# A fused attention and feed-forward kernel: first pair's queries and keys in two sets, one transfer for a pair's value windows, later feed-forward weight loads

## The chip, the cores and the metric

The kernel runs on one core of one Trainium2 chip. The metric is the device time of one execution in microseconds (us); less is better. Three runs of the kernel before took 882.73, 882.87 and 884.77 us, median 882.87 us.

## The reference

Inputs are q, k, v of shape (4, 8, 576, 64) and two pairs of feed-forward weights, (512, 2048) and (2048, 512), with two scalars s and b.

```python
# attention, per batch and head; scale = 1/8, factor = 4
q_d, k_d, v_d = means over groups of 4 positions            # 144 positions
out_d   = softmax(scale * q_d @ k_d.T) @ v_d, each row repeated 4 times
mask    = abs(pos_i - pos_j) < 4                            # band of 7
out_loc = softmax(where(mask, scale * q @ k.T, -1e9)) @ v
x = (out_d repeated + out_loc), laid out as (2304 tokens, 512)
# layer 1: h = x @ w_in;  g = h if h > 0 else exp(h) - 1;  x = g @ w_out
# layer 2: h = x @ w_in;  g = s * relu(h)**2 + b;          out = g @ w_out
```

## The kernel before, in words

The program has two stages: attention over 16 pairs of heads (four batches, four pairs `u` in each; pairs are numbered 0 to 15 below), and two feed-forward layers of 24 slots each. Each engine has its program written out in order, and semaphores join them.

**Attention.** Four buffers (slots) hold the inputs of four pairs. `qbd` holds the queries of a pair block-diagonally: head 0 in partitions 0 to 63, head 1 in 64 to 127, and zeros in the other half, which are written once. `kall` holds the keys. `vwin` holds the values as nine overlapping windows of 70 rows, one for each tile of 64 queries; `v4` holds them by groups of four positions for the pooled branch. For a pair,

- TensorE (PE) computes `scores` (L475: nine tiles of 64 queries against their windows of 70 keys, two heads, 18 products; tiles 0 to 4 go to one PSUM bank and 5 to 8 to another), `dscores` (L484, pooled), `turn` in four groups (L499 and L503, transposes of the probabilities) and `values` (L519 band, L528 pooled).
- VectorE (DVE) computes `pool_k` (L923), `mask` (L930, scale and add the band, one instruction for each bank), `max_band` (L938), `max_pooled` (L943, L947), the two `normalise` steps (L954, L956, L965, L973), and adds the two branches into `xy` (L1100).
- ScalarE (ACT) computes the exponentials (`exp_band` L674, tile by tile; `exp_pooled` L684), and copies the transposes (L761 to L771) and the pooled result (L781) out of PSUM. It zeroes the padding of slots 1 to 3 at the start (L744; slot 0 is done by DVE, L916).
- GpSimd (POOL) builds the identity and the band mask, then does `pool_q` (L434, L436) and `pool_v` (L441, L443).
- SyncE (SP) issues every DMA. `load_qk` issues one DMA for the keys (L289) and two for the queries (L293); `load_v` issues six for `vwin` (L300 to L305) and one for `v4` (L306).

The engines' programs are software-pipelined. On PE a step `i` runs `dscores(i+1)`, the first two groups of `turn(i)`, `scores(i+2)`, the last two groups, `values(i)`. On DVE the order ahead of the loop is `pool_k(0)`, `mask(0)`, `max_band(0)`, `pool_k(1)`, `max_pooled(0)`, `mask(1)`, `max_band(1)`, `normalise_band(0)`, `normalise_pooled(0)`. On POOL a step `i` waits for the probabilities of pair `i+1` and runs `pool_q(i+3)` and `pool_v(i+1)`. On SP a step `i` loads the queries and keys of pair `i+4` when pair `i` has been read, then the values of pair `i+3` when `values_ready` has counted `i+1` (it starts at 1, so the values of pair `i-1` are done). The helper `pairs` runs the first two batches as a hardware loop of four pairs and writes the last two out. `left` counts down to 0 over the pairs that are written out: in the kernel before, the first weights of the feed-forward layers (512 KB each, into `wstage`) are issued at pairs 11 (`left == 4`), 12 and 13.

**Feed-forward.** 48 slots, each of three-term products of split fp32 operands: into `ps_h` (L552 for the first two slots, L603 for the others) and into `ps_y` (L632 in layer 1, L639 in layer 2). The first product `tile(0, 0)` stands before the values of pair 15 on PE. ACT and DVE split the operands (L714, L995 for the first weights) and evaluate the activation.

Of the kernel before, what the change touches and what calls it, by code (L numbers as in the profile page):

```python
# [18 lines left out]
ALU = mybir.AluOpType  # L19
# [3 lines left out]
AX_X = mybir.AxisListType.X  # L23
# [1 line left out]
P = 128  # L25


def attention_moe_moe2(nc, q_t, k_t, v, w_in0, w_out0, w_in1, w_out1, s, b, out):
    B, H, D, S = q_t.shape
    TOK, DM = out.shape  # L30
    POOL = 4
# [13 lines left out]
    SCALE = float(D) ** -0.5  # L45
# [30 lines left out]
    RAW = (0, 1) + tuple(range(2, FP)) + (FP + 2, FP + 3) + tuple(range(NB * FP, (NB + 1) * FP))  # L76
    FETCHED = tuple(sl for sl in range(SLOTS) if sl not in RAW)

    NV = 7
    E_CREDIT = 2  # L80

    with ExitStack() as whole:
        def sem(name):
            return whole.enter_context(nc.semaphore(name))
# [57 lines left out]
        k_loaded = [sem(f"k_loaded{i}") for i in range(CH)]  # L142
        v_loaded = [sem(f"v_loaded{i}") for i in range(CH)]
        w_loaded = [[sem(f"w_{x}_loaded{i}") for i in range(2)] for x in ("in", "out")]
        sb_loaded = sem("sb_loaded")

        pads_zero = sem("pads_zero")
        slots_zero = sem("slots_zero")
        consts_ready = sem("consts_ready")
        pool_order = sem("pool_order")  # L150
        dve_order = sem("dve_order")
# [46 lines left out]

        def pairs(eng, body):

            with eng.Fori(0, B - 2) as n:
                for u in range(CH):
                    body(n, u, PAIRS)
            for n in range(B - 2, B):
                for u in range(CH):
                    body(n, u, PAIRS - 1 - (n * CH + u))

# [79 lines left out]
        def _(sp):  # L287
            def load_qk(bb, slot):
                sp.dma_start(kall[:, slot, :],  # L289
                             k_t[bb, 2 * slot:2 * slot + 2].rearrange("h d s -> (h d) s")).then_inc(k_loaded[slot], 16)  # L290
                for h in range(2):
                    rows = slice(h * D, (h + 1) * D)
                    sp.dma_start(qbd[rows, slot, h, :], q_t[bb, 2 * slot + h]).then_inc(q_loaded[slot], 16)  # L293

            def load_v(bb, slot):
                vp = v[bb, slot]
                inner = vp[QT - REACH:QT - REACH + (NT - 2) * QT].rearrange("(t r) x -> r t x", r=QT)
                rest = vp[2 * QT - REACH:2 * QT - REACH + (NT - 2) * QT].rearrange("(t r) x -> r t x", r=QT)
                dst = vwin[:, slot].rearrange("p t h d -> p t (h d)")
                sp.dma_start(dst[0:QT, 1:NT - 1, :], inner).then_inc(v_loaded[slot], 16)  # L300
                sp.dma_start(dst[QT:WIN, 1:NT - 1, :], rest[0:2 * REACH]).then_inc(v_loaded[slot], 16)
                for t in (0, NT - 1):
                    a = WSTART[t]
                    sp.dma_start(dst[0:QT, t, :], vp[a:a + QT]).then_inc(v_loaded[slot], 16)
                    sp.dma_start(dst[QT:WIN, t, :], vp[a + QT:a + WIN]).then_inc(v_loaded[slot], 16)  # L305
                sp.dma_start(v4[:, slot].rearrange("p k i x -> p k (i x)"),  # L306
                             vp.rearrange("(k p i) x -> p k (i x)", k=2, i=POOL)
                             ).then_inc(v_loaded[slot], 16)

            def load_w_in(sl):  # L310

                i = RAW.index(sl)
                if i >= 2:
                    sp.wait_ge(w_split[0], i - 1)
                sp.dma_start(wstage[i % 2][:, 0, :], (w_in0, w_in1)[layer_of(sl)][:, pair_of(sl), :]).then_inc(w_loaded[0][i % 2], 16)

            def load_w_out(sl):

                if sl >= 2:
                    sp.wait_ge(w_split[1], sl - 1)  # L320
                sp.dma_start(wstage[sl % 2][:, 1, :], (w_out0, w_out1)[layer_of(sl)][:, pair_of(sl), :]).then_inc(w_loaded[1][sl % 2], 16)
# [14 lines left out]
                    sp.dma_start(wc[x][:, sl % 2].rearrange("p k x -> p (k x)").bitcast(F32),  # L336
                                 wc_kept[layer_of(sl), pair_of(sl), x]).then_inc(wc_loaded[sl % 2], 16)

            load_qk(0, 0)
            load_qk(0, 1)  # L340
            load_v(0, 0)
            load_qk(0, 2)
# [6 lines left out]
            def step(n, u, left):  # L349
                i = n * CH + u  # L350
                if left >= CH:
                    sp.wait_ge(scores_ready, i + 1)
                    sp.wait_ge(q_pooled, i + 1)
                    sp.wait_ge(k_pooled, i + 1)
                    load_qk(n + 1, u)
                if left >= 3:
                    sp.wait_ge(values_ready, i + 1)
                    load_v(n + (u + 3) // CH, (u + 3) % CH)
                if left == 4:
                    load_w_in(0)  # L360
                if left == 3:
                    load_w_out(0)
                if left == 2:
                    load_w_in(1)
                    load_w_out(1)
            pairs(sp, step)

# [29 lines left out]
        def _(pool):  # L397
# [40 lines left out]
            def pool_v(n, u):  # L438
# [11 lines left out]
            pool.wait_ge(slots_zero, 2 * (CH - 1))  # L450

            pool.wait_ge(dscores_ready, 1)
            pool_q(0, 2)
# [12 lines left out]

        @block.tensor
        def _(pe):
            def scores(n, u):
                pe.wait_ge(k_loaded[u], 16 * (n + 1))  # L470
                pe.wait_ge(q_loaded[u], 32 * (n + 1))
                for t in range(NT):
# [4 lines left out]
                mm.then_inc(scores_ready, 1)  # L477

            def dscores(n, u):
                i = n * CH + u  # L480
# [80 lines left out]
            pe.wait_ge(slots_zero, 2 * (CH - 1))  # L561
            scores(0, 1)
            pe.wait_ge(consts_ready, 1)

            def step(n, u, left):
                i = n * CH + u
                if left >= 1:
                    pe.wait_ge(exp_ready, 2 * i + 2)
                    dscores(n + (u + 1) // CH, (u + 1) % CH)
                turn(n, u, 0)  # L570
                turn(n, u, 1)
                if left >= 2:
                    pe.wait_ge(masked, i + 2)
                    scores(n + (u + 2) // CH, (u + 2) % CH)
# [91 lines left out]
        def _(act):  # L666
            act.sem_inc(turn_copied, E_CREDIT)

            def exp_band(n, u, tiles):
                i = n * CH + u  # L670
                act.wait_ge(negmax_ready, 2 * i + 1)
                for t in tiles:
                    x = prob[:, u, t, :]
                    ins = act.activation(x, x, ACT.Exp, bias=stat[:, u % 2, 1, t:t + 1],  # L674
                                         accum_out=stat[:, u % 2, 2, t:t + 1])
                if t == NT - 1:
                    ins.then_inc(exp_ready, 1)
# [72 lines left out]
            first_tiles, last_tiles = range(0, NTX), range(NTX, NT)  # L750
            exp_band(0, 0, range(NT))
            exp_pooled(0, 0)
            exp_band(0, 1, first_tiles)

            def step(n, u, left):
# [24 lines left out]
                act.wait_ge(dvalues_ready, i + 1)  # L780
                act.activation(xd[:], ps_xd[:, 0:SD], ACT.Copy).then_inc(xd_copied, 1)  # L781
                if left >= 2:
                    exp_band(n2, u2, first_tiles)
                if left == 3:
                    hi_quarter(0, 0)
# [125 lines left out]
        def _(dve):  # L911
# [146 lines left out]
                dve.tensor_tensor(x_source(blk, k), a, z, op).then_inc(x_sum, 1)  # L1058

            dve.wait_ge(dve_order, 2)  # L1060
            pool_k(0, 0)
# [198 lines left out]
```

## Time and profile before

| what | us |
|---|---|
| median of three runs | 882.87 |
| the profiled execution | 881.78 |
| its span | 880.0 |
| PE busy | 856.6 (97%) |
| DVE busy | 621.4 (71%) |
| ACT busy | 449.2 (51%) |
| POOL busy | 65.5 (7%) |
| DMA queue q1, share of 16 engines' span | 50.0% |

Times in the profile are from the start of the span. Busy shares are means over both stages: POOL works in the attention stage only, and ACT is almost full there. The profile lists, for an instruction or a merged run of equal instructions, its start, its length and, in brackets, how long its engine had been idle and what ended that.

### The profile page before, as it was taken

The numbers are of one execution on the slowest core, as the hardware profiler recorded it, in microseconds if no ns is written. First come the engines' busy times: TensorE is split into PE (matmuls) and PEld (weight loads), VectorE is DVE, ScalarE is ACT, GpSimd is POOL, SyncE is SP. The second block draws the span as 40 slices with busy tenths as digits, with TensorE's granted clock in tenths as the row PEclk, the third lists the DMA queues.
The fourth block names the chain that finished last, engine by engine and source line by source line (L and its number), as shares of the span: only waits on it lengthen the run. The fifth ranks groups of instructions, "written<-read, shape, count | busy, mean of one in ns | idle before, by whom it ended". The sixth has DMA issues, their size and how long they took to land.

```text
span 880.0 us, 14879 instructions
## 1 busy us (share of the span) xinstructions
PE 856.6 (97%) x5660; PEld 779.9 (89%) x5660; DVE 621.4 (71%) x976; ACT 449.2 (51%) x928; POOL 65.5 (7%) x84
## 2 busy tenths in 40 slices
PE   5999899999999999999999999999999999999998
PEld 5888799999989999999999898998899888898897
DVE  6999887787776666755667887787755658655464
ACT  7999976545655344453445553434423235232332
POOL 5656410000000000000000000000000000000000
PEclk9999999999999999999999999999999999999999
DMA  8879925545525434354352554635554435535321
GB/s 193 205 178 203 202 76 199 196 156 199 206 97 214 170 125 174 133 176 147 116 207 72 206 172 156 233 133 197 208 181 153 170 108 191 203 136 187 108 84 72
DMA packets 44192, 143.94 MB, mean 164 GB/s; under 512 B 5120, under 2 KB 15200, under 8 KB 44128
## 3 DMA queue, kind: packets, MB, share of 16 engines
q1 hardware_dynamic: 44128, 143.07, 50.0%
q8 instruction: 42, 0.69, 0.3%
q14 instruction: 22, 0.18, 0.1%
HBM read 108.97 MB, written 34.08 MB: 163 GB/s over the span
## 4 chain that ended last, share of the span: by engine, by line
PE 86%; DVE 4%; POOL 3%; issue 3%; ACT 2%; DMA 2%; SPq 1%; POOLq 0%; DVEq 0%; ACTq 0%
PE ps_h L603 37%; PE ps_y L639 22%; PE ps_y L632 21%; PE ps_h L552 2%; DMA qbd<-in_qt 2%; POOL v L441 1%; PE ps_t L499 1%; POOL q_half L434 1%; PE ps_s L475 1%; ACT prob L674 1%; PE ps_sd L484 1%; DVE hsum L1110 1%; PE ps_xd L528 1%; DVE xs_lo L981 1%; POOL vd L443 1%
## 5 line engine op out<-in xcount | busy, mean ns | idle before, releaser
L1110 DVE TENSOR_TENSOR hsum<-hsum,ps_h 128x384 f32<-128x384 f32 x322 | 176.9, 551 | 167.0 <-PE ps_h L603 164.3
L603 PE MATMUL ps_h<-xs_hi,wc_hi 128*128 128x384 f32 x644 | 218.8, 340 | 1.8 <-DVE hsum L1110 1.6
L603 PE MATMUL ps_h<-xs_lo,wc_hi 128*128 128x384 f32 x644 | 217.4, 338 | 0.0
L603 PE MATMUL ps_h<-xs_hi,wc_lo 128*128 128x384 f32 x644 | 217.3, 337 | 0.0
L825 ACT ACTIVATE act_out<-act_out,sb 128x768 f32<-128x768 f32 x48 | 49.5, 1031 | 228.6 <-DVE act_out L1125 228.6
L603 PEld LDWEIGHTS ps_h<-xs_hi,wc_hi 128*128 128x128 f32 x644 | 121.0, 188 | 12.1 <-issue 1.5
L603 PEld LDWEIGHTS ps_h<-xs_lo,wc_hi 128*128 128x128 f32 x644 | 121.0, 188 | 8.8
L1131 DVE TENSOR_TENSOR g_lo<-act_out,g_hi 128x768 fp32r<-128x768 f32 x96 | 91.6, 954 | 49.6 <-ACT g_hi L836 49.6
L603 PEld LDWEIGHTS ps_h<-xs_hi,wc_lo 128*128 128x128 f32 x644 | 121.0, 188 | 0.0
L639 PE MATMUL ps_y<-wo_hi,g_hi 128*128 128x512 f32 x288 | 113.0, 392 | 1.5 <-ACT xsum L846 1.5
L639 PE MATMUL ps_y<-wo_hi,g_lo 128*128 128x512 f32 x288 | 113.9, 395 | 0.0
L639 PE MATMUL ps_y<-wo_lo,g_hi 128*128 128x512 f32 x288 | 113.0, 392 | 0.0
L632 PE MATMUL ps_y<-g_hi,wo_hi 128*128 128x512 f32 (+1 forms) x384 | 98.7, 338 | 0.0
L632 PE MATMUL ps_y<-g_hi,wo_lo 128*128 128x512 f32 (+1 forms) x384 | 97.8, 336 | 0.0
L632 PE MATMUL ps_y<-g_lo,wo_hi 128*128 128x512 f32 (+1 forms) x384 | 97.8, 336 | 0.0
L836 ACT ACTIVATE g_hi<-act_out 128x768 fp32r<-128x768 f32 x96 | 80.9, 843 | 30.0 <-DVE act_out L1118 29.3
L816 ACT ACTIVATE act_out<-hsum 128x768 f32<-128x768 f32 x48 | 40.6, 845 | 108.9 <-DVE hsum L1110 108.9
L632 PEld LDWEIGHTS ps_y<-g_lo,wo_hi 128*128 128x128 f32 x384 | 65.5, 188 | 8.7
L632 PEld LDWEIGHTS ps_y<-g_hi,wo_lo 128*128 128x128 f32 x384 | 65.4, 188 | 8.0
L632 PEld LDWEIGHTS ps_y<-g_hi,wo_hi 128*128 128x128 f32 x384 | 68.5, 188 | 2.2
L639 PEld LDWEIGHTS ps_y<-wo_hi,g_lo 128*128 128x128 f32 x288 | 54.0, 187 | 12.3
L639 PEld LDWEIGHTS ps_y<-wo_hi,g_hi 128*128 128x128 f32 x288 | 54.1, 188 | 8.7 <-issue 2.1
(91 smaller groups left out, 1094.6 us busy)
## 6 DMA issues: line engine op xcount, KB each, us to landing
wc_hi<-wc_kept SPq DMA_DIRECT2D x30, 896.0 KB, 4.5
wc_lo<-wc_kept SPq DMA_DIRECT2D x30, 896.0 KB, 6.4
wstage<-in_w_out SPq DMA_DIRECT2D x48, 512.0 KB, 3.5
wc_kept<-wc_hi SPq DMA_DIRECT2D x16, 896.0 KB, 3.6
wc_kept<-wc_lo SPq DMA_DIRECT2D x16, 896.0 KB, 6.3
wstage<-in_w_in SPq DMA_DIRECT2D x18, 512.0 KB, 7.1
kall<-in_kt SPq DMA_DIRECT2D x16, 288.0 KB, 4.5
qbd<-in_qt SPq DMA_DIRECT2D x32, 144.0 KB, 4.5
```

Source lines behind the costliest of these rows:

```text
L434: pool.tensor_tensor(q_half[:, u % 2], x[:, :, 0:2], x[:, :, 2:4], ALU.add).then_inc(q_part, 1)
L441: pool.tensor_tensor(x[:, :, 0:2, :], x[:, :, 0:2, :], x[:, :, 2:4, :], ALU.add).then_inc(v_part, 1)
L443: pool.tensor_tensor(vd[:, u % 2], x[:, :, 0, :], x[:, :, 1, :], ALU.add).then_inc(v_pooled, 1)
L552: mm = pe.matmul(o, wc[a][:, sl % 2, W_QUARTER[k, f], c * P:(c + 1) * P], xs[x][:, X_AT[r, k], c, :], start=(q == 0 and k == 0 and c == 0) ...
L603: mm = pe.matmul(o, wc[a][:, sl % 2, W_SLOT[k], c * P:(c + 1) * P], xs[x][:, X_SLOT[k], c, :], start=(c == 0 and q == 0), stop=(c == 1 and ...
L632: mm = pe.matmul(ps_yf[:, o:o + end - start], wo[a][:, sl % 2, f, u * P:(u + 1) * P], g[x][:, sl % 2, f, start:end], start=(first and q == ...
L639: mm = pe.matmul(ps_y[:, m, :], g[a][:, sl % 2, f, m * P:(m + 1) * P], wo[x][:, sl % 2, f, :], start=(first and q == 0), stop=(last and q ...
L816: act.activation(x, hsum[:, sl % 2, f, :], ACT.Relu, scale=-1.0).then_inc(relu_ready, 1)
L825: act.activation(x, x, ACT.Identity, bias=sb[:, 1:2], scale=sb[:, 0:1]).then_inc(affine_ready, 1)
L836: act.activation(g[0][:, sl % 2, f, :], act_out[:, f, :], ACT.Copy).then_inc(hi_ready, 1)
L1110: dve.tensor_tensor(part(sl, *out_at), part(sl, *in_at), ps_h[:, prod_number(sl, pos) % 2, 0:TH], op).then_inc(h_added, 1)
L1131: dve.tensor_tensor(g[1][:, sl % 2, f, :], act_out[:, f, :], g[0][:, sl % 2, f, :].bitcast(F32), ALU.subtract).then_inc(g_ready, 1)
```

## The change

Four things change.

1. The first pair's queries and keys come in two sets. The first set has the columns that tiles 0 to 4 need (320 queries of each head, 323 keys), the second the rest. PE's `scores(0)` runs as two parts, DVE's `mask(0)` and `max_band(0)` as two parts with semaphores of their own, and ACT's exponentials of tiles 0 to 4 start after the first part. DVE's `pool_k(0)` moves behind the first part of the maximum.
2. The nine value windows of a pair are laid out in the input by the host, and one DMA of 70 rows of 4608 bytes replaces six; with `v4` a pair's values take two DMAs in place of seven.
3. The zeroing of slot 3's padding moves from ACT to POOL (two memsets, ahead of `pool_q(0)`).
4. `pairs` loops over three batches and writes only the last one out. The first feed-forward weights are issued at pairs 13, 14 and 15, each behind a wait for the values of the pair before the last.

The waits for loaded queries and keys move out of `scores`, and the wait for the maximum out of `exp_band`, to their callers.

```diff
-    NV = 7
+    NV = 2
...
-            with eng.Fori(0, B - 2) as n:
+            with eng.Fori(0, B - 1) as n:
                 for u in range(CH):
                     body(n, u, PAIRS)
-            for n in range(B - 2, B):
-                for u in range(CH):
-                    body(n, u, PAIRS - 1 - (n * CH + u))
+            for u in range(CH):
+                body(B - 1, u, CH - 1 - u)
...
             def load_v(bb, slot):
                 vp = v[bb, slot]
-                inner = vp[QT - REACH:QT - REACH + (NT - 2) * QT].rearrange("(t r) x -> r t x", r=QT)
-                rest = vp[2 * QT - REACH:2 * QT - REACH + (NT - 2) * QT].rearrange("(t r) x -> r t x", r=QT)
-                dst = vwin[:, slot].rearrange("p t h d -> p t (h d)")
-                sp.dma_start(dst[0:QT, 1:NT - 1, :], inner).then_inc(v_loaded[slot], 16)
-                sp.dma_start(dst[QT:WIN, 1:NT - 1, :], rest[0:2 * REACH]).then_inc(v_loaded[slot], 16)
-                for t in (0, NT - 1):
-                    a = WSTART[t]
-                    sp.dma_start(dst[0:QT, t, :], vp[a:a + QT]).then_inc(v_loaded[slot], 16)
-                    sp.dma_start(dst[QT:WIN, t, :], vp[a + QT:a + WIN]).then_inc(v_loaded[slot], 16)
+                sp.dma_start(vwin[:, slot].rearrange("p t h d -> p (t h d)"), v_t[bb, slot]).then_inc(v_loaded[slot], 16)
...
-            load_qk(0, 0)
+            cut_q, cut_k = NTA * QT, WSTART[NTA - 1] + WIN
+            k_first = k_t[0, 0:2].rearrange("h d s -> (h d) s")
+            sp.dma_start(kall[:, 0, 0:cut_k], k_first[:, 0:cut_k]).then_inc(k_early, 16)
+            for h in range(2):
+                sp.dma_start(qbd[h * D:(h + 1) * D, 0, h, 0:cut_q], q_t[0, h, :, 0:cut_q]).then_inc(q_early, 16)
+            sp.dma_start(kall[:, 0, cut_k:], k_first[:, cut_k:]).then_inc(k_loaded[0], 16)
+            for h in range(2):
+                sp.dma_start(qbd[h * D:(h + 1) * D, 0, h, cut_q:], q_t[0, h, :, cut_q:]).then_inc(q_loaded[0], 16)
...
-                if left == 4:
+                if left == 2:
+                    sp.wait_ge(values_ready, i + 1)
                     load_w_in(0)
-                if left == 3:
+                if left == 1:
+                    sp.wait_ge(values_ready, i + 1)
                     load_w_out(0)
-                if left == 2:
                     load_w_in(1)
+                if left == 0:
+                    sp.wait_ge(values_ready, i + 1)
                     load_w_out(1)
...
+            for h in range(2):
+                pool.memset(qbd[h * D:(h + 1) * D, CH - 1, 1 - h, :], 0.0).then_inc(last_slot_zero, 1)
+            pool.wait_ge(last_slot_zero, 2)
             pool.wait_ge(pads_zero, 2)
+            pool.wait_ge(q_early, 32)
             pool_q(0, 0)
...
             pe.wait_ge(pads_zero, 2)
-            scores(0, 0)
+            pe.wait_ge(k_early, 16)
+            pe.wait_ge(q_early, 32)
+            scores(0, 0, range(0, NTA), scores_early)
+            pe.wait_ge(k_loaded[0], 16)
+            pe.wait_ge(q_loaded[0], 32)
+            scores(0, 0, range(NTA, NT), scores_ready)
             dscores(0, 0)
...
-            for slot in range(1, CH):
+            for slot in range(1, CH - 1):
...
-            exp_band(0, 0, range(NT))
+            act.wait_ge(negmax_early, 1)
+            exp_band(0, 0, first_tiles)
+            act.wait_ge(negmax_ready, 1)
+            exp_band(0, 0, last_tiles)
             exp_pooled(0, 0)
+            act.wait_ge(negmax_ready, 3)
             exp_band(0, 1, first_tiles)
...
+            mask_part(0, first_tiles).then_inc(masked_early, 1)
+            dve.wait_ge(masked_early, 1)
+            max_part(first_tiles).then_inc(negmax_early, 1)
             pool_k(0, 0)
-            dve.wait_ge(consts_ready, 3)
-            mask(0, 0)
-            max_band(0, 0)
+            dve.wait_ge(scores_ready, 1)
+            mask_part(1, last_tiles).then_inc(masked, 1)
+            dve.wait_ge(masked, 1)
+            max_part(last_tiles).then_inc(negmax_ready, 1)
             pool_k(0, 1)
```

## Rows read from the trace of the kernel before

**Rows 1.** The page, chain that ended last: shares of the span by engine.

```profile
PE 86%; DVE 4%; POOL 3%; issue 3%; ACT 2%; DMA 2%; SPq 1%; POOLq 0%; DVEq 0%; ACTq 0%
```

**Rows 2.** Windows: stretch, its length, PE, PEld, DVE, ACT, POOL busy (instructions), clock, DMA.

```profile
14.00:17.50 3.50, 3.02 (x14) 2.78 (x14) 3.08 (x7) 2.24 (x13) 2.38 (x2) 0.51 0.99 220
20.00:94.00 74.00, 68.52 (x1228) 61.27 (x1225) 68.89 (x169) 72.98 (x362) 44.63 (x48) 1.00 0.87 193
94.00:102.50 8.50, 6.90 (x135) 6.20 (x129) 7.54 (x19) 8.37 (x41) 4.42 (x5) 1.00 1.06 189
102.50:106.50 4.00, 4.00 (x25) 3.18 (x21) 3.76 (x9) 3.57 (x15) 1.99 (x2) 0.57 1.08 208
109.50:113.00 3.50, 3.50 (x32) 2.61 (x26) 3.01 (x6) 2.83 (x8) 2.04 (x2) 0.52 0.13 52
117.00:880.00 763.00, 756.41 (x4035) 691.33 (x4032) 521.82 (x745) 341.42 (x435) 0.00 (x0) 1.00 0.45 160
```

**Rows 3.** Timeline, first 18 us: start, length, engine, line, operation, idle before and releaser.

```profile
1.19 1.19 SPq L293 DMA_DIRECT2D qbd<-in_qt  x2
3.06 1.11 SPq L293 DMA_DIRECT2D qbd<-in_qt  x2
5.78 2.37 PE L475 MATMUL ps_s<-kall,qbd 128*64 128x70 f32 x36 [5.78 <-DMA qbd<-in_qt]
7.03 0.67 POOL L436 TENSOR_TENSOR qd<-q_half 128x288 f32<-128x288 f32 x1
8.07 1.75 PE L484 MATMUL ps_sd<-kd,qd 128*96 128x144 f32 x6
9.76 1.74 PE L475 MATMUL ps_s<-kall,qbd 128*64 128x70 f32 x36
10.02 0.35 ACT L674 ACTIVATE prob<-prob,stat 128x70 f32<-128x70 f32 x1 [3.27 <-DVE stat L938]
13.64 0.82 DVE L965 TENSOR_TENSOR prob<-prob,stat 128x630 f32<-128x630 f32 x1
14.48 1.73 PE L484 MATMUL ps_sd<-kd,qd 128*96 128x144 f32 x6 [2.99 <-ACT probd L684]
16.00 1.77 PE L499 MATMUL ps_t<-ident,prob 128*70 128x128 f32 x8
17.18 0.59 ACT L761 ACTIVATE probt<-ps_t 70x512 f32<-70x512 f32 x1 [1.26 <-PE ps_t L499]
```

**Rows 4.** Timeline, the same work on PE after 20 us.

```profile
21.81 0.95 PE L484 MATMUL ps_sd<-kd,qd 128*96 128x144 f32 x6
23.56 1.33 PE L475 MATMUL ps_s<-kall,qbd 128*64 128x70 f32 x36
```

**Rows 5.** Instructions of L293, the queries' transfers: time to landing.

```profile
DMA to landing us min/median/max: 3.2/4.5/9.4
```

**Rows 6.** Windows in the first transfers: keys on 128 partitions, then a half of queries.

```profile
2.50:3.25 0.75, 0.00 (x0) 0.00 (x0) 0.17 (x2) 0.73 (x2) 0.69 (x4) 1.00 1.01 390
3.50:4.50 1.00, 0.00 (x0) 0.00 (x0) 0.61 (x1) 0.96 (x2) 0.95 (x6) 1.00 0.79 148
```

**Rows 7.** Waits of the DMA-issuing queue, 0 to 150 us: total, times, longest us.

```profile
SPq L300 <- PE ps_x L519: 1.4, 2, 1.2
```

**Rows 8.** Timeline, last pairs of the attention.

```profile
87.41 1.11 SPq L293 DMA_DIRECT2D qbd<-in_qt  x2
97.46 1.15 POOL L434 TENSOR_TENSOR q_half<-qbd 128x576 f32<-128x576 f32 x1 [2.81 <-DMA qbd<-in_qt]
101.53 0.72 PE L528 MATMUL ps_xd<-probdt,vd 72*64 72x144 f32 x8 [1.05 <-POOL vd L443]
109.65 1.07 ACT L714 ACTIVATE wc_hi<-wstage 128x1024 fp32r<-128x1024 f32 x1
```

**Rows 9.** The page, DMA issues: KB each, median us to landing.

```profile
wstage<-in_w_out SPq DMA_DIRECT2D x48, 512.0 KB, 3.5
wc_hi<-wc_kept SPq DMA_DIRECT2D x30, 896.0 KB, 4.5
```

More of the change, by code:

```diff
@@ L25, with attention_moe_moe2 @@
 P = 128
-def attention_moe_moe2(nc, q_t, k_t, v, w_in0, w_out0, w_in1, w_out1, s, b, out):
+def attention_moe_moe2(nc, q_t, k_t, v, v_t, w_in0, w_out0, w_in1, w_out1, s, b, out):
     B, H, D, S = q_t.shape
@@ L144, in attention_moe_moe2 @@
         w_loaded = [[sem(f"w_{x}_loaded{i}") for i in range(2)] for x in ("in", "out")]
+        k_early = sem("k_early")
+        q_early = sem("q_early")
+        scores_early = sem("scores_early")
+        masked_early = sem("masked_early")
+        negmax_early = sem("negmax_early")
         sb_loaded = sem("sb_loaded")
@@ L148, in attention_moe_moe2 @@
         slots_zero = sem("slots_zero")
+        last_slot_zero = sem("last_slot_zero")
         consts_ready = sem("consts_ready")
@@ L449, in _ @@
             pool_v(0, 0)
-            pool.wait_ge(slots_zero, 2 * (CH - 1))
+            pool.wait_ge(slots_zero, 2 * (CH - 2))
             pool.wait_ge(dscores_ready, 1)
@@ L468, in _, with scores @@
         def _(pe):
[L469 to L472, printed above, removed]
+            def scores(n, u, tiles, done):
+                for t in tiles:
                     bank, a = (0, t * WIN) if t < NTA else (1, (t - NTA) * WIN)
@@ L476, in scores @@
                                        kall[:, u, WSTART[t]:WSTART[t] + WIN], start=True, stop=True)
-                mm.then_inc(scores_ready, 1)
+                mm.then_inc(done, 1)
             def dscores(n, u):
@@ L557, in _ @@
             pe.wait_ge(pads_zero, 2)
-            scores(0, 0)
+            pe.wait_ge(k_early, 16)
[4 more added lines that the diff above has]
+            scores(0, 0, range(NTA, NT), scores_ready)
             dscores(0, 0)
             pe.wait_ge(masked, 1)
-            pe.wait_ge(slots_zero, 2 * (CH - 1))
-            scores(0, 1)
+            pe.wait_ge(slots_zero, 2 * (CH - 2))
+            pe.wait_ge(last_slot_zero, 2)
+            pe.wait_ge(k_loaded[1], 16)
+            pe.wait_ge(q_loaded[1], 32)
+            scores(0, 1, range(NT), scores_ready)
             pe.wait_ge(consts_ready, 1)
@@ L573, in step @@
                     pe.wait_ge(masked, i + 2)
-                    scores(n + (u + 2) // CH, (u + 2) % CH)
+                    n2, u2 = n + (u + 2) // CH, (u + 2) % CH
+                    pe.wait_ge(k_loaded[u2], 16 * (n2 + 1))
+                    pe.wait_ge(q_loaded[u2], 32 * (n2 + 1))
+                    scores(n2, u2, range(NT), scores_ready)
                 turn(n, u, 2)
@@ L670, in exp_band @@
                 i = n * CH + u
-                act.wait_ge(negmax_ready, 2 * i + 1)
                 for t in tiles:
@@ L782, in step @@
                 if left >= 2:
+                    act.wait_ge(negmax_ready, 2 * i + 5)
                     exp_band(n2, u2, first_tiles)
@@ L1060, in _, with mask_part, max_part @@
             dve.wait_ge(dve_order, 2)
+            dve.wait_ge(k_early, 16)
+            dve.wait_ge(scores_early, 1)
+            dve.wait_ge(consts_ready, 3)
+            first_tiles, last_tiles = slice(0, NTA), slice(NTA, NT)
+            def mask_part(bank, tiles):
+                part = prob[:, 0, tiles, :]
+                count = tiles.stop - tiles.start
+                return dve.scalar_tensor_tensor(out=part, in0=ps_s[:, bank, 0:count * WIN].rearrange("p (t w) -> p t w", w=WIN),
+                                                scalar=SCALE, in1=band[:, tiles, :], op0=ALU.mult, op1=ALU.add)
+            def max_part(tiles):
+                return dve.tensor_reduce(stat[:, 0, 1, tiles], prob[:, 0, tiles, :], AX_X, ALU.max, negate=True)
+            mask_part(0, first_tiles).then_inc(masked_early, 1)
+            dve.wait_ge(masked_early, 1)
+            max_part(first_tiles).then_inc(negmax_early, 1)
             pool_k(0, 0)
-            dve.wait_ge(consts_ready, 3)
-            mask(0, 0)
-            max_band(0, 0)
+            dve.wait_ge(scores_ready, 1)
+            mask_part(1, last_tiles).then_inc(masked, 1)
+            dve.wait_ge(masked, 1)
+            max_part(last_tiles).then_inc(negmax_ready, 1)
             pool_k(0, 1)
@@ L1238, in lay_w_out, with lay_v_tiles @@
         return np.ascontiguousarray(x.transpose(2, 0, 1, 3)).reshape(128, w.shape[0] // 256, 2 * w.shape[1])
+    def lay_v_tiles(x):
+        tiles = [x[:, :, a:a + 70] for a in [min(max(t * 64 - 3, 0), x.shape[2] - 70) for t in range(x.shape[2] // 64)]]
+        y = np.stack(tiles, axis=3)
+        return np.ascontiguousarray(y).reshape(*y.shape[:3], -1)
     nc = bacc.Bacc("TRN2", target_bir_lowering=False, num_devices=1)
+    pairs_of_v = np.ascontiguousarray(v.reshape(v.shape[0], v.shape[1] // 2, 2, *v.shape[2:]).transpose(0, 1, 3, 2, 4)).reshape(
+        v.shape[0], v.shape[1] // 2, v.shape[2], 2 * v.shape[3])
     arrays = {
@@ L1243 @@
         "in_kt": np.ascontiguousarray(k.transpose(0, 1, 3, 2)),
-        "in_v": np.ascontiguousarray(v.reshape(v.shape[0], v.shape[1] // 2, 2, *v.shape[2:]).transpose(0, 1, 3, 2, 4)).reshape(
-            v.shape[0], v.shape[1] // 2, v.shape[2], 2 * v.shape[3]),
+        "in_v": pairs_of_v,
+        "in_v_tiles": lay_v_tiles(pairs_of_v),
         "in_w_in0": lay_w_in(moe_w_in),
```

## The prediction

> **What bounds the kernel now.** I read the page's chain first. It is PE for 86% of the span, with small shares for everything else, DMA 2% among them [rows 1], so what this change can win lies in the few microseconds in which the chain is not PE's. The windows by stage say where those are. From 117 us to the end PE is busy for 756.4 of 763 us with DMA at 0.45 [rows 2]: a feed-forward stage that only starts earlier or later as a block. From 20 to 94 us ACT is busy for 72.98 of 74 us. POOL has 48 instructions there at four a pair, so these are 12 pairs at 6.17 us each, and the change takes no instruction from ACT in any of them. All that can move are the first 18 us, the tail from 94 to 117 us, and DMA if it should become a bound. Then I read the timeline of the first 18 us [rows 3] and of the tail [rows 8]; the reader should look at the idle time in brackets and ask who ends it.
>
> **The values in two transfers.** It takes five DMA issues a pair from SP. SP's queue waited for work only twice in 150 us, 1.4 us in all [rows 7]: it issues back to back and runs behind. After the change it gets ahead and waits for values instead. Nobody downstream waited for it before 94 us, since ACT is full [rows 2], so the gain there is 0. The bytes of the windows are the same 9 x 70 rows of 512 bytes (322 KB), now in 70 rows of 4608. Cost bounds: a key transfer on 128 partitions moved at 390 GB/s, a half of the queries on 64 partitions at 148 GB/s [rows 6]. 322 KB take 0.8 us at the one and 2.2 us at the other. A pair's other loads are keys (295 KB, 0.8 us), queries (2 x 147 KB at 148 GB/s, 2.0 us) and `v4` (295 KB, 0.8 to 2.0 us). The sum is 4.4 to 7.0 us against 6.17 us a pair. Today's kernel already moves those bytes in smaller pieces at a share of 0.87 [rows 2], that is 5.4 us a pair, and long rows do well elsewhere (896 KB in rows of 7 KB land in 4.5 us, 199 GB/s with all latency in it [rows 9]). I take 5 us, under the pair's time: 0. The Trainium skill ("SBUF — State Buffer", on the DMA port swizzle) says that a transfer to 64 partitions reaches only half of the ports; the trace agrees (148 against 390 GB/s), and by that rule the 70 long rows, which lie almost wholly in the first 64 partitions, go no faster than the small pieces did, so fewer descriptors do not double their rate.
>
> **The hardware loop over three batches.** A pair costs the same in the loop and written out (the 12 pairs at 6.17 us cross from one to the other at 64 us, with ACT full throughout [rows 2]): 0, at most 0.2 us at one more loop end.
>
> **The first pair in two sets.** Before, the second half of the queries is issued at about 1.8 us [rows 3] and PE starts at 5.78 us. Of the first set the same transfer has 80 KB for 144. The shortest landing of a query transfer is 3.2 us [rows 5], so it lands at 1.8 + 3.2 = 5.0 us (at the earliest 4.6, if the 64 KB that are left out save 0.4 us at 148 GB/s [rows 6]; at the latest just before 5.78, as before); PE starts about 5.1. The 20 early products take 20/36 of 2.37 us, 1.3 us, to 6.4. From the end of `scores(0)` (5.78 + 2.37 = 8.15) mask and maximum took until 10.02, 1.9 us; 5/9 of it is 1.0. So the exponentials start at about 7.5 us instead of 10.02, a lead of 2.5 us.
>
> What becomes of this lead? ACT next needs the first transposes of pair 0 (17.18 us, after 1.26 us idle [rows 3]), and these hang on another chain. The second set's last transfer is issued where that of pair 1 was, at about 3.6 us [rows 3], and lands at 3.6 + 3.2 = 6.8 us (at latest like pair 1's, whose `pool_q` began at 7.9). `pool_q(0)` wants the whole of the queries: it took from 5.80 to 7.70 (1.15 us for the first half as at 97.46 [rows 8], then 0.67 [rows 3]) and now ends at 6.85 + 1.9 = 8.75. `dscores(0)` therefore starts at about 8.8 us, where it started at 8.07. That is **0.7 us later**, and behind it stand, in PE's order, `scores(1)`, and in DVE's, mask, maximum and `normalise_band(0)`. From the start of `dscores(0)` to the end of `normalise_band(0)` it was 14.46 - 8.07 = 6.4 us [rows 3], so the first transpose can start at 15.2 us. Before, it started at 16.00, not at 14.46, because PE had taken up `dscores(1)`, which waited for the pooled exponentials until 14.48 and then ran for 1.5 us. Those exponentials now end about 2 us sooner, at some 12.3 us, so `dscores(1)` slips into the gap and is gone by the time. Gain: 16.0 - 15.2 = **0.8 us** of the 2.5.
>
> The clock adds to it. PE had been idle from 11.5 to 14.4 us, and its granted clock was 0.51 from 14.0 to 17.5 us [rows 2], the lower of its two levels (1.2 GHz). `dscores` took 1.73 us there, and 0.95 at the upper one [rows 3, 4]. With the idle stretch broken up the fall may come later or not at all: up to 0.5 us on the four transposes that ACT waits for (half of 1.18 us), to 0; I take 0.2. The products before 10 us, too, ran at half pace (2.37 and 1.75 us against 1.33 and 0.95 [rows 3, 4]); were they all at full pace, `dscores(0)` and `scores(1)` would take 2.3 us for 3.4, another 1.1 us. An earlier start with holes in it makes that no likelier: 0. The start gives **1.0 us** in all, between -0.3 (second set as late as 7.85 us) and 2.4 (both clock terms in full, cut a little).
>
> The Trainium skill ("TensorE: Matmul & The Clock Gate", What's actually happening) has it that the low rate is the default and activity releases it. The row agrees: the first products run at half pace. That rule speaks against cutting PE's first work in two; the time it gives stands among the rivals, worked out from rows.
>
> **The padding on POOL.** Two memsets of 64x576 stand ahead of `pool_q(0)` on POOL. Before, POOL's `pool_q(0)` began right at the landing, about 5.8 us (7.03 less 1.15 and a step [rows 3]); now it waits for the second set until 6.8, so the two memsets have at least that 1 us. If they took 1 us each, POOL would be up to 1 us late, and the forecast's gain of 0.8 gone; a memset moves no more than half the bytes of an operation that takes 1.15 us on 128x576, so I take 0. ACT's zeroing shrinks by 1.3 us in a stretch in which it waits anyway.
>
> **The weights held.** Before, the queries of pair 15 are issued at 87.41 us and POOL idles 2.81 us for them until 97.46 [rows 8], with DMA at a share of 1.06 [rows 2]. SP, ahead by now, will issue them up to 9 us sooner: this wait goes whether the weights are held or not. What was it worth? About 0.7 us later than POOL's usual beat; PE had 1.05 us idle at 101.53 for it [rows 8]; but ACT was busy for 8.37 of the 8.5 us [rows 2], and ACT sets the beat. So directly 0. What is late next is ACT, with the extra copies of the feed-forward inputs in its program. Indirectly the clock: it fell to the lower level from 102.5 to 106.5 and from 109.5 to 113 us [rows 2], and ACT lost 0.43 and 0.67 us in these two (idle: 4.00 - 3.57 and 3.50 - 2.83). One or both falls may go. As ACT still makes PE wait, I take 0.2 us, between -0.5 and 1.1. The holding itself costs: weight 0 is asked for after the values of pair 12, about 96 us, and used at 109.65 [rows 8]; 512 KB land in 3.5 us in the median [rows 9], so 10 us of cover are left. The next two are asked for at about 103 us and used from 117 us on, the fourth at about 110 us and used later still; each has more than 7 us. If a cover failed, every microsecond would be on the path, since `tile(0, 0)` waits for weight 0.
>
> **Sum.** 1.0 + 0.2 = 1.2 us off the profiled execution's 881.78 us (880.0 of span and 1.78 around it), 880.6. The median of the three runs is 1.09 us above this execution, so as a median: 882.87 - 1.2 = **881.7 us**.
>
> **Rivals.**
> (a) *The whole lead goes through.* If `dscores(0)` is not what binds (the second set lands with the first, and the clock rises before 10 us), then 2.5 us come from the start, and the tail's falls of the clock go too: 0.6. 879.8 us. For it: 2.5 us are there on ACT. Against it: `pool_q(0)` needs all columns.
> (b) *The lead is lost.* The second set lands at 7.85 us like pair 1's did; then `dscores(0)` is 1.7 us late, transposes start at 16.2, and the rest is nothing: 882.9 us. For it: 4.5 us is the median landing [rows 5], and the share of DMA is full there.
> (c) *The clock, slower.* PE's first work now has holes of 0.4 and 0.9 us. It stays at the lower level through `scores(1)` (2.37 for 1.74, 0.6 us), and when the fall of 14.0 us comes two microseconds later it covers `scores(2)` and the transposes ahead of it (1.0 + 0.2). With (b)'s loss of 0.2 that is 2.0 us slower, 884.9 us; alone, against the forecast's 0.8, 883.9 us. It decides from the point at which the clock is still low at 11 us and low again at 17.5. Against it: idle stretches get shorter in sum.
> (d) *DMA is the bound.* If a pair's transfers take 7.0 us, 13 pairs lose 0.8 us each: 893 us. Against it: 5.4 us today with smaller pieces.
>
> **How the numbers follow.** Chances: forecast 0.60, (a) 0.15, (b) 0.15, (c) 0.06, (d) 0.04. A measurement of this kernel can tell 0.3%, 2.65 us, from no change. Of the cases only (a), with its clock terms in full, reaches 880.2: faster 0.15 with some of the forecast's far end. Slower than 885.5 are (d) and a bad (c): 0.06. Same 0.79. The range leaves out (d) and the ends of (a) and (c): 879.6 to 883.8.
>
> **What the profile after would show.** Right: `scores` start at 5.1 us, exponentials at 7.5, `dscores(0)` near 8.8, the first transpose near 15.2 and ACT's copy near 16; pairs still 6.2 us apart; SP's queue waiting for values in every pair; no wait of POOL for the last queries, and the feed-forward products from about 115.8 us. The forecast is wrong if the first transposes come before 14.5 or after 16.2 us, if a pair takes anything but 6.1 to 6.2 us, or if ACT's idle time in the tail changes by more than 1 us.

## The result and the profile after

The changed kernel takes 890.09 us in the median of 15 runs (883.76 to 897.13), the kernel before 883.56 us in 15 runs beside it (880.30 to 885.22). The ratio is 1.0070 (95% interval 1.0052 to 1.0087): 6.5 us **slower** by the medians, where 1.2 us of gain was forecast. (The ratio leaves out the run of 897.13 us, over 1.5% above the fastest.) The spread has grown from 5 us to 13 us; the profiled execution, at 896.84 us (span 895.0), lies near its upper end, so its lengths overstate the usual loss.

The windows of the changed kernel, in the columns of [rows 2], show where the 15 us are that the span of this execution is longer than before (895.0 against 880.0):

```profile
0.00:20.00 20.00, 11.47 (x114) 9.65 (x116) 11.09 (x24) 12.34 (x45) 12.47 (x30) 1.00 0.84 174
20.00:40.00 20.00, 14.30 (x242) 12.28 (x239) 14.40 (x34) 14.07 (x70) 7.54 (x9) 0.92 0.96 173
40.00:60.00 20.00, 19.01 (x254) 16.75 (x250) 14.63 (x36) 15.86 (x78) 9.66 (x11) 0.76 0.89 189
60.00:94.00 34.00, 31.67 (x541) 27.93 (x541) 28.43 (x71) 31.47 (x155) 18.17 (x20) 0.94 0.86 197
132.00:895.00 763.00, 756.44 (x4037) 691.33 (x4033) 521.82 (x744) 341.47 (x436) 0.00 (x0) 1.00 0.45 160
```

The feed-forward stage is untouched: the last 763 us have PE busy for 756.44 us, as in [rows 2] with 756.41. The attention stage is longer, and in it ACT, which was busy for 72.98 of 74 us, is busy for only 14.07 of 20 us between 20 and 40 us. The instruction counts tell the pace: 9 on POOL from 20 to 40 us, a little over two pairs in the time of three. DMA meanwhile is almost full, 0.96 at 173 GB/s. Most of the loss is early: the pooled values of pair 3 start at 49.24 us where they started at 39.45, those of pair 8 at 84.05 (70.33), those of pair 15 at 130.97 (115.92). So 9.8 of the 15 us are lost by pair 3.

The start, in the columns of [rows 3]:

```profile
4.29 1.43 PE L485 MATMUL ps_s<-kall,qbd 128*64 128x70 f32 x20 [4.29 <-DMA qbd<-in_qt]
6.09 1.20 PE L485 MATMUL ps_s<-kall,qbd 128*64 128x70 f32 x16 [0.37 <-DMA qbd<-in_qt]
8.06 1.75 PE L494 MATMUL ps_sd<-kd,qd 128*96 128x144 f32 x6 [0.77 <-POOL qd L444]
10.83 2.37 PE L485 MATMUL ps_s<-kall,qbd 128*64 128x70 f32 x36 [1.01 <-DMA qbd<-in_qt]
16.97 1.92 PE L509 MATMUL ps_t<-ident,prob 128*70 128x128 f32 x8 [2.09 <-DVE prob L990]
```

The two sets work better than forecast (scores from 4.29 us for 5.1, pooled scores from 8.06 for 8.8; before, 5.78 and 8.07). Then PE waits 1.01 us for the queries of pair 1, which the forecast did not have; the first transposes come at 16.97 us instead of 16.00.

What happened shows in SP's own timeline (start, length, operation):

```profile
12.00 0.37 SPq L304 DMA_DIRECT2D v<-in_v  x1
14.15 1.16 SPq L299 DMA_DIRECT2D qbd<-in_qt  x2
17.87 5.08 SPq L299 DMA_DIRECT2D qbd<-in_qt  x2
24.93 2.62 SPq L299 DMA_DIRECT2D qbd<-in_qt  x2
```

The landing times of the queries' transfers that are issued up to 60 us (line L299, without the first pair), and the longest entry of what SP's queue waited for up to 150 us:

```profile
DMA to landing us min/median/max: 3.1/12.1/19.0
```

```profile
SPq L303 <- PE ps_x L529: 47.7, 12, 7.7
```

SP has all of the first four pairs' queries and keys and three pairs' values under way by 12.4 us (before: by 18.4 us), and the queries of pairs 4 and 5 by 23 us. At 17.87 us even its issuing stalls: two issues take 5.08 us where they take 1.16. The median landing of a query transfer goes from 4.3 us before, in the same 60 us (4.5 over all pairs [rows 5]), to 12.1 us. From then on SP waits for the values in nearly every pair (47.7 us in 12 waits; 1.4 us in 2 before [rows 7]): whatever slot comes free is refilled at once. Most loads were asked for earlier and took longer to land. In the chain of work that ended last (start, length, what), the longest wait for a load is that for the second half of pair 3's queries, and the longest other wait is a stop of PE:

```profile
10.75 15.08 DMA qbd<-in_qt
34.93 3.33 issue
```

The waits up to 125 us (engine, line, what it waited for: us in total, times, longest) name who pays:

```profile
POOL q_half L442 <- DMA qbd<-in_qt: 9.4, 3, 5.9
PE ps_s L485 <- DMA qbd<-in_qt: 6.5, 4, 4.3
PE ps_t L513 <- issue: 3.3, 1, 3.3
PE ps_s L485 <- issue: 1.4, 1, 1.4
```

Of PE's 6.5 us for queries, 4.3 are the start, which was 5.8 us before. Two kinds of wait are new. Queries come late: POOL waits 5.88 us for those of pair 3, where in the kernel before no such wait was longer than 2.8 us ([rows 8]). And PE stands still where it waits for nothing that the profile knows, 1.38 us in the middle of the 36 products of one `scores` and 3.33 us between two transposes:

```profile
28.09 0.83 PE L485 MATMUL ps_s<-kall,qbd 128*64 128x70 f32 x19 [1.38 <-issue]
38.27 1.18 PE L513 MATMUL ps_t<-ident,probd 96*72 96x96 f32 x6 [3.33 <-issue]
```

In the window 34 to 38.5 us the code queues move one block each:

```profile
q8 instruction: 1, 0.02, 2.1%
q14 instruction: 1, 0.01, 0.9%
```

So one reading is that PE waits for its own code, which travels on the same DMA engines. The evidence is thin: in the kernel before, q8 also moves one block from 34 to 38.5 us, and PE does not stop. The Trainium skill ("Runtime: NRT & Kernel Launch", Instruction fetch mechanics) says that a sequencer fetches its next block of code through a DMA queue of its own, and calls the cost mostly hidden; here a stop is there to see, but no row ties it to a block. After the stop of 3.33 us the granted clock is at the lower level, 0.50 from 37 to 44 us (1.2 GHz), and PE's work takes longer still:

```profile
37.00:44.00 7.00, 5.73 (x56) 5.35 (x57) 2.71 (x6) 3.93 (x20) 2.13 (x4) 0.50 0.83 168
```

### The profile page after: what moved, and what is told of

Same layout as the page of the kernel before. It is cut to its first block, busy times and chain, and to the rows that moved or that the text cites. A ratio compares the mean times of both kernels' runs of the same rounds, so it can differ in the third digit from the quotient of the medians.

```text
span 895.0 us, 14879 instructions
## 1 busy us (share of the span) xinstructions
PE 866.0 (97%) x5660; PEld 787.1 (88%) x5660; DVE 621.8 (69%) x977; ACT 448.9 (50%) x926; POOL 67.9 (8%) x86
## 4 chain that ended last, share of the span: by engine, by line
PE 86%; DVE 4%; issue 3%; ACT 2%; POOL 2%; DMA 2%; SPq 1%; POOLq 0%; DVEq 0%; ACTq 0%
PE ps_h L624 36%; PE ps_y L660 22%; PE ps_y L653 21%; PE ps_h L562 2%; DMA qbd<-in_qt 2%; PE ps_t L509 1%; PE ps_s L485 1%; PE ps_sd L494 1%; PE ps_x L529 1%; PE ps_xd L538 1%; DVE hsum L1153 1%; POOL v L449 1%; ACT prob L694 1%; POOL q_half L442 1%; DVE xs_lo L1006 1%
```

## The experiments

Theory A, *run-ahead*: with five fewer issues a pair SP no longer paces itself, and sends transfers far ahead; near loads and code wait among them. Theory B: rows of 4608 bytes are slower on the wire. Rival C: the two sets, the longer loop or the held weights cost the time. All ratios are to the kernel before on the same chip.

| kernel | median us (range) | ratio (95%) |
|---|---|---|
| changed kernel | 890.09 (883.76 to 897.13) | 1.0070 (1.0052 to 1.0087) |
| rows_only | 887.88 (882.81 to 893.34) | 1.0063 (1.0029 to 1.0097) |
| one_dma_short_rows | 888.50 (883.89 to 894.85) | 1.0068 (1.0042 to 1.0094) |
| sets_and_hold | 884.27 (881.86 to 885.62) | 1.0006 (0.9993 to 1.0019) |
| sets_only | 883.65 (881.39 to 894.09) | 1.0018 (0.9993 to 1.0043) |
| hold_only | 882.98 (881.62 to 886.05) | 1.0000 (0.9986 to 1.0015) |
| paced | 884.41 (882.70 to 886.74) | 1.0016 (1.0002 to 1.0030) |
| paced_loop | 885.24 (881.41 to 887.10) | 1.0014 (0.9998 to 1.0030) |
| paced_start | 885.64 (882.82 to 892.79) | 1.0034 (1.0012 to 1.0057) |
| thin_v | 885.68 (882.62 to 889.15) | 1.0047 (1.0029 to 1.0065) |
| rows_paced | 881.95 (879.78 to 885.50) | 0.9997 (0.9983 to 1.0011) |
| hold_paced_rows | 882.96 (880.40 to 885.96) | 1.0010 (0.9998 to 1.0023) |

The kernel before had medians of 883.33 us (beside rows_only, sets_and_hold, one_dma_short_rows and paced), 883.25 us (beside paced_start, paced_loop, sets_only and hold_only) and 882.37 us (beside the other three).

**Which part.** rows_only is the kernel before with the values' two transfers:

```diff
-                inner = vp[QT - REACH:QT - REACH + (NT - 2) * QT].rearrange("(t r) x -> r t x", r=QT)
...
-                    sp.dma_start(dst[QT:WIN, t, :], vp[a + QT:a + WIN]).then_inc(v_loaded[slot], 16)
+                sp.dma_start(vwin[:, slot].rearrange("p t h d -> p (t h d)"), v_t[bb, slot]).then_inc(v_loaded[slot], 16)
```

> The kernel before with one edit: a pair's nine value windows come in one transfer of 70 rows of 4608 bytes instead of six transfers. Theory A (run-ahead: fewer issues let SP put far more transfers in flight, and the near loads and code loads wait among the far ones): slower than before by 5 to 8 us, 888 to 891 us, with landings of queries of 10 us and more in the first 40 us. Theory B (the form of the long rows lowers the rate of the transfers): the same time, 888 to 891 us. Rival C (the cut first pair, the longer hardware loop or the held weights are what costs): within 2 us of before.

sets_and_hold is the changed kernel with this one edit undone.

> The changed kernel with the six window transfers of before put back; the two sets of the first pair, the padding on POOL, the loop over three batches and the held weights stay. Theories A and B: 881 to 883.5 us, as the forecast had it for these parts (1.2 us under before). Rival C: 888 us or more.

The transfer of the values alone brings 0.63% (interval 0.29 to 0.97), most or all of the loss, and the wide range with it; without it both are gone. Rival C falls. The forecast for the other parts (a gain) does not come either. In sets_and_hold the pooled values of pair 0 run at 19.14 us, where they ran at 20.55. SP is three issues later than before and asks for the queries of pair 4 only at 22.28 us (before: 20.16); POOL takes them up at 28.77, no later than before (28.99), so this by itself loses nothing. But PE, ahead of the others, was busy for only 2.7 of 4 us from 24 to 28, and then its clock is low:

```profile
26.67 1.03 PE L546 MATMUL ps_xd<-probdt,vd 72*64 72x144 f32 x8 [1.32 <-POOL vd L459]
28.77 1.15 POOL L450 TENSOR_TENSOR q_half<-qbd 128x576 f32<-128x576 f32 x1 [2.25 <-DMA qbd<-in_qt]
28.00:31.00 3.00, 3.00 (x22) 2.70 (x19) 1.68 (x5) 1.70 (x11) 2.15 (x3) 0.50 0.86 228
```

The pooled values of pair 1 are still 0.5 us ahead (26.67 against 27.22); those of pair 2, at 35.51 us (before: 33.08), are behind. The parts by themselves are sets_only, which adds the changes to the first pair to the kernel before, and hold_only, which adds the longer loop and the held weights:

```diff
-            load_qk(0, 0)
+            sp.dma_start(kall[:, 0, 0:cut_k], k_first[:, 0:cut_k]).then_inc(k_early, 16)
...
```

```diff
-            with eng.Fori(0, B - 2) as n:
+            with eng.Fori(0, B - 1) as n:
-                if left == 4:
+                if left == 2:
+                    sp.wait_ge(values_ready, i + 1)
                     load_w_in(0)
...
```

> The kernel before with the first pair in two sets and the padding on POOL alone. The forecast's step gave 1.0 us of gain (882.3 us by a before of 883.3). By what sets_and_hold showed (the values of pair 0 come 1.4 us sooner, then the queries of pair 4 come late behind SP's own issues and the clock falls): within 1 us of before.

> The kernel before with the hardware loop over three batches and the first feed-forward weights held. The forecast's step: 0.2 us of gain with bounds of -0.5 to 1.1. If holding starves the feed-forward stage or a third turn of the loop costs: 1 us or more slower.

Neither is told from before. The third turn of the loop and the held weights cost nothing that shows, as forecast; the gain of 1.0 us that the start was to bring did not show. One of the twelve runs of sets_only took 894.09 us, without the long transfer; no trace of that run is kept, so what held it up is not known.

**Rows or run-ahead.** one_dma_short_rows keeps the single issue but lays the windows out tile by tile, so that the transfer consists of 630 rows of 512 bytes:

```diff
-sp.dma_start(vwin[:, slot].rearrange("p t h d -> p (t h d)"), v_t[bb, slot])
+sp.dma_start(vwin[:, slot].rearrange("p t h d -> p t (h d)"), v_t[bb, slot].rearrange("t r x -> r t x"))
```

> The changed kernel, but the windows are laid out tile by tile in memory, so that the one transfer of a pair's windows has 630 rows of 512 bytes, as many short rows as before, and still one issue. Theory A (number of issues): as slow as the changed kernel, 887 to 892 us, with landings above 10 us. Theory B (length of the rows): back at 881 to 883.5 us.

As slow as the changed kernel, 1.0068. The trace has nearly twice the packets of the changed kernel in the first 60 us (10174 for 5423), median landings are 9.6 us for queries and 11.9 for keys, and PE stops at the same instruction as in the changed kernel, the first transpose of the pooled probabilities of pair 2, for 1.88 us. The length of the rows makes no difference here; theory B falls. paced keeps the long rows and holds SP back, with two waits ahead of the loop (the start brake) and one in it (the loop brake):

```diff
+            sp.wait_ge(scores_ready, 1)
             load_qk(0, 2)
             load_v(0, 1)
+            sp.wait_ge(probs_ready, 1)
             load_qk(0, 3)
...
                 if left >= CH:
+                    sp.wait_ge(dvalues_ready, i + 1)
                     sp.wait_ge(scores_ready, i + 1)
```

> The changed kernel with its long rows, but SP is held back to about the pace of before: the loads of pair 2 wait for the first scores, those of pair 3 for the first normalised probabilities, and in the loop the queries and keys of pair i+4 for the pooled values of pair i. Theory A: 881 to 884 us, landings of queries back at 4 to 6 us. Theory B: 887 us or more, since every transfer is as slow as it was.

884.41 us, and the range is back to 4 us. Three waits, and nothing else, take back 5.7 of the 6.5 us by the medians, or 0.54 of the 0.70% by the ratios. The 0.16% that is left (0.02 to 0.30) is small and not explained by any run. The median landing of queries is 3.8 us between 20 and 40 us. The windows of 20 to 94 us, for paced, rows_only and one_dma_short_rows in this order, are worth a look:

```profile
20.00:94.00 74.00, 68.16 (x1214) 60.90 (x1212) 68.55 (x168) 72.36 (x358) 43.59 (x47) 1.00 0.77 196
20.00:94.00 74.00, 68.32 (x1210) 60.98 (x1210) 68.05 (x168) 71.91 (x356) 42.83 (x46) 1.00 0.92 208
20.00:94.00 74.00, 64.87 (x1139) 57.60 (x1138) 65.67 (x159) 68.52 (x336) 41.11 (x44) 0.99 0.97 189
```

The rate is about the same, but the share of DMA is 0.77 where SP is held back and 0.92 to 0.97 where it is not. So the share is no measure of how much room is left: about the same bytes at about the same rate show 0.77 or 0.92 and more, by how much stands in the queue.

**Where the run-ahead costs.** The two brakes one at a time:

```diff
+            sp.wait_ge(scores_ready, 1)
             load_qk(0, 2)
             load_v(0, 1)
+            sp.wait_ge(probs_ready, 1)
             load_qk(0, 3)
```

for paced_start, and for paced_loop

```diff
                 if left >= CH:
+                    sp.wait_ge(dvalues_ready, i + 1)
```

> The changed kernel with SP held back only before the loop (pair 2 behind the first scores, pair 3 behind the first normalised probabilities). Where does the run-ahead cost? If the burst of the first 12 us does it: 884 to 885 us, as with both brakes. If it is the loop, in which a slot is refilled the moment it is free: 888 us or more. I expect about half, 886 to 887 us.

> The changed kernel with SP held back only in the loop (queries and keys of pair i+4 wait for the pooled values of pair i). The first four pairs are issued within 13 us as in the changed kernel. If the burst at the start is the cost: 888 us or more; if the loop is: 884 to 885 us.

The loop brake alone does as much as both (1.0014 and 1.0016). The start brake alone does about half (1.0034): the queue builds up in the loop instead, with median landings of 14.9 us for queries between 20 and 40 us and 17.2 us between 60 and 90. My guess of half fits the start brake by its ratio (its 885.64 us lie just under the 886 to 887); for the loop brake the run, at 885.24 us, comes closest to the second alternative, 884 to 885. The intervals of paced_start and paced_loop overlap, so that the loop matters more is likely and no more.

thin_v takes the brakes off again and loads less from pair 4 on:

```diff
+                if thin:
+                    sp.dma_start(vwin[:, slot, 0:4].rearrange("p t h d -> p (t h d)"), v_t[bb, slot, :, 0:4 * P]).then_inc(v_loaded[slot], 16)
+                    sp.dma_start(v4[:, slot, 0].rearrange("p i x -> p (i x)"), vp[0:POOL * KD].rearrange("(p i) x -> p (i x)", i=POOL)).then_inc(v_loaded[slot], 16)
+                    return
```

> The changed kernel with SP unbraked and its long rows, but from pair 4 on only four of a pair's nine value windows and half of v4 are loaded (0.87 MB a pair instead of 1.20; the rest keeps the values of an earlier pair, which changes the result). The theory now: the transfers need about all that the DMA engines give (1.20 MB per 6.17 us is 194 GB/s; the changed kernel moves 188 to 190 at a share of 0.9), so what SP sends ahead stands in the queue and never drains. Then with 27% less the queue drains within some pairs and the time is 881 to 884 us, landings of queries under 6 us after 60 us. If sending ahead itself were the cost, whatever the load: 887 us or more.

885.68 us: the forecast of 881 to 884 missed, and so did 887 or more (the kernel before took 882.37 us in this set). The trace shows why. The queue of thin_v drains by 40 us (median landing of queries 13.0 us from 20 to 40 us, 3.9 from 40 to 60, 3.4 from 60 to 90), and from then on a pair takes 5.9 to 6.5 us, 6.2 in the mean. The loss is made before:

```profile
20.00:40.00 20.00, 16.53 (x266) 14.54 (x266) 16.06 (x40) 16.14 (x81) 8.11 (x9) 0.96 0.94 198
40.00:60.00 20.00, 18.57 (x343) 16.52 (x340) 18.63 (x46) 19.84 (x97) 12.46 (x14) 1.00 0.68 165
60.00:90.00 30.00, 27.25 (x475) 24.30 (x471) 27.91 (x69) 29.16 (x147) 18.24 (x21) 1.00 0.47 140
```

ACT is at 16.14 of 20 us between 20 and 40 us and at 19.84 between 40 and 60. So sending ahead costs time while the first pairs are being filled, whatever the later load; and with less to load the queue drains afterwards. With the full load (1.21 MB in 6.17 us is 196 GB/s, within the 173 to 220 that these kernels move with a full queue) it need not: from 60 to 90 us the median landing of queries is still 17.2 us in paced_start and 10.1 in rows_only. In the changed kernel's own trace it does fall, from 17.9 us (20 to 40 us) to 10.6 (40 to 60) and 5.7 (60 to 90), but this execution had lost most of its time by then, and pairs that take longer ask for less. A long queue is a risk rather than a loss of its own: the profiled execution of rows_only took only 883.25 us with it, others of its runs up to 893.34. What was asked for early enough comes in time even after 10 us; an engine stops where the request was late for the queue that it met.

**A version without the loss.** rows_paced is the kernel before with the long rows and both brakes, hold_paced_rows has the held weights and the longer loop as well.

> The kernel before with the long rows alone, and both brakes on SP. Run-ahead theory: the rows cost nothing by themselves, 882.5 to 884 us, same as before, against 887.9 without brakes. If long rows are slower transfers in themselves: 885 us or more.

> Candidate for a version at least as good as both: rows_paced with the held weights and the loop over three batches, without the two sets. ACT sets the beat of a pair, so nothing but the tail can gain: 882 to 883.5 us, not told from before.

rows_paced is at 0.9997: with SP held back, long rows cost nothing that shows, and gain nothing; ACT, busy for 72.03 of 74 us, sets the pace of a pair as before. Its window:

```profile
20.00:94.00 74.00, 68.56 (x1220) 61.16 (x1217) 68.60 (x168) 72.03 (x357) 43.34 (x47) 1.00 0.77 194
```

No version here beats the kernel before by more than its interval.

## Why the prediction was wrong, by its own steps

- **The step that failed** is "The values in two transfers": "After the change it gets ahead and waits for values instead. Nobody downstream waited for it before 94 us, ... so the gain there is 0." That SP would get ahead was right (47.7 us of waiting). That getting ahead is free was the mistake: the term was put at 0 and measured 0.63% in rows_only, 4.6 us by the medians. I asked only who waited for SP, not what SP's slowness held back. The brakes show it: paced, with three waits on SP, is at 1.0016, and rows_paced at 0.9997. The kernel before had a sign of it: the queries that it issued at 87.41 us stood with 512 KB weight loads, landed after up to 9.4 us ([rows 5]), and POOL waited 2.81 us for them [rows 8]. I took that for SP being late, and missed that the queue was long.
- The signs named for a wrong forecast came: the first transposes at 16.97 us (limit 16.2), the pooled values of pairs 1 and 2 10.1 us apart (30.36 and 40.49 us) for 6.2, the feed-forward products in one block from 132 us for 115.8.
- **The DMA sum** (4.4 to 7.0 us a pair, 5 us taken) was asked the wrong question. The rate did suffice: paced and rows_paced move all bytes at the pace of a pair. It also read the share of 0.87 as 5.4 us of work out of 6.17, with room above it; but the same bytes show a share of 0.77 in paced and 0.92 in rows_only. Rival (d), with a chance of 0.04 and a price of 10 us, took DMA for the bound because a pair's bytes need 7.0 us; paced and rows_paced, with a pair in 6.2 us, refute that. The range ended at 883.8 because (d), the only case with a DMA loss, was left out of it.
- **The first pair in two sets.** Landings of small transfers were over-priced (2.3 to 2.6 us for 3.2): scores at 4.29 us (forecast 5.1), pooled scores at 8.06 (8.8). The transfers of pair 1 are issued 1.8 us later (4.86 for 3.06) and meet the queue: `scores(1)` starts at 10.83 us. Without the run-ahead it starts as early as before (9.76), but it takes 2.37 us for 1.74. In sets_and_hold, then in paced:

```profile
9.67 2.37 PE L493 MATMUL ps_s<-kall,qbd 128*64 128x70 f32 x36
15.18 1.06 PE L517 MATMUL ps_t<-ident,prob 128*70 128x128 f32 x8 [1.59 <-DVE prob L998]
```

```profile
15.59 1.44 PE L512 MATMUL ps_t<-ident,prob 128*70 128x128 f32 x8 [2.20 <-DVE prob L993]
16.95 2.37 PE L488 MATMUL ps_s<-kall,qbd 128*64 128x70 f32 x36
```

  The first transposes come at 15.18 us, in sets_only at 15.25, where 15.2 was forecast: the 0.8 us are there. But luck has a part in it. `dscores(0)` starts 0.8 us sooner than forecast, and the chain behind it, taken as a fixed 6.4 us, is about 0.8 us longer; two errors cancel. And the gain does not last: in sets_only the pooled values of pair 0 start at 20.46 us, 0.1 us ahead of before, in paced at 20.89, 0.3 us behind.
- **The clock** takes most of it back: in sets_only `scores(2)`, behind the transposes, takes 1.92 us for 1.33. Rival (c), given 0.06, had this mechanism: `scores(1)` takes its 2.37 us in the changed kernel, paced and sets_and_hold, and in paced the fall comes about two microseconds later than before (0.50 from 17 to 19 us, where it was 0.51 from 14.0 to 17.5) and covers `scores(2)`, 2.37 us for 1.33. In sets_and_hold the clock does not fall before 20 us, and pair 0 is 1.4 us ahead; it falls later. In the changed kernel the clock is low from 37 to 47 us and again near 58 to 61, 71 to 75 and 122 to 129 us, but not after PE's stop at 28 us. Before 20 us its clock row reads 1.00 throughout, while lengths such as 2.37 us are those of the lower level, so there the lengths decide.
- **Loop and held weights**: 0 for the loop and 0.2 us for the weights; hold_only, at 1.0000 (0.9986 to 1.0015), cannot tell either from nothing. The wait of POOL for the last queries is gone in the changed kernel; that it is worth nothing, as forecast, agrees with hold_only.
- **What stays open** is how the 6 us divide among late queries, stops that look like code loading, and the clock that follows both. The stop at the pooled transposes of pair 2 is in the traces of four kernels without the loop brake (3.33 us, 1.88 in one_dma_short_rows, 2.13 in thin_v, 1.25 in paced_start) and in none with it, but no run removed it alone. In sets_only POOL waits for queries too (7.4 us in 3 waits), PE makes no such stop, and no loss clear of the interval shows. That the stops are code loads is a guess from the code queues' rows, not shown.

## What to carry to other kernels

A slow issuing queue can be the brake that keeps the DMA queue short. Before making loads cheaper to issue, work out the bytes per step over the step's time and compare them with the rate moved in a stretch where landings are already long (here 196 GB/s wanted, 173 to 220 moved); in any other stretch the rate shown is only what was asked for. Where the two are close, tie each prefetch to a semaphore of the consumer, here the loads of pair i+4 to the pooled values of pair i, or the loads needed next will stand behind those needed later. Judge DMA by time to landing, not by its busy share.

## What the runs showed of the hardware

- With demand near the rate, sending ahead took the median landing of 144 KB from 3.4 to 3.8 us (paced, 20 to 90 us) to 14.9 to 17.2 us (paced_start, same stretch, by windows), and the rate did not rise with it (195 to 199 against 173 to 186 GB/s).
- The issuing engine stalls too: in the changed kernel two issues took 5.08 us (at 17.87 us) and 2.62 us (at 24.93), for 1.16 at 14.15.
- 630 rows of 512 bytes and 70 rows of 4608 bytes made no difference in time (1.0068 against 1.0070).
- PE can stop for 1.2 to 3.3 us where no wait shows, between independent instructions, while DMA is full; in four kernels it was the same instruction (3.33, 1.88, 2.13 and 1.25 us). The cause is not shown.
- The DMA share depends on the queue and not on the rate alone: 0.77 at 196 GB/s (paced), 0.92 at 208 (rows_only), 0.97 at 189 (one_dma_short_rows).
